# Linear-attention recurrence feeding a mixture of experts: state products on quarters of TensorE's array, and the low halves of w3 on GpSimd

## What is computed

```python
f = 1.0 / (1.0 + np.exp(-f_logit))          # q, k, v, f_logit: (4, 8, 768, 48)
for t in range(S):
    state = f[:, :, t, :, None] * state + np.einsum('bhd,bhe->bhde', k[:, :, t], v[:, :, t])
    y[:, :, t] = np.einsum('bhd,bhde->bhe', q[:, :, t], state)
```

## Time and profile before

| | us |
|---|---|
| median of three runs (728.39 to 729.1) | 728.86 |
| profiled execution | 729.75 |
| its span in the trace | 728.0 |
| end of the recurrence in the trace | 148.9 |
| TensorE busy | 714.8 |
| VectorE busy | 350.7 |
| ScalarE busy | 290.2 |
| GpSimd busy | 200.3 |

### The profile page before, as it was taken

How to read it: one execution, slowest core, us unless ns; L and a number is a source line. 1 busy time by engine, 2 the same in 40 slices (tenths; PEclk the granted TensorE clock), 3 DMA queues, 4 the chain that set the end, 5 groups by cost and what they waited for, 6 DMA issues and landing times.

```text
span 728.0 us, 14063 instructions
## 1 busy us (share of the span) xinstructions
PE 714.8 (98%) x4911; PEld 655.6 (90%) x4911; DVE 350.7 (48%) x580; ACT 290.2 (40%) x557; POOL 200.3 (28%) x234
## 2 busy tenths in 40 slices
PE   7999999999989999999999999999999999999997
PEld 6999899989989999999999988988988989889887
DVE  6889998768745545455465541211312113112121
ACT  5677788534235534345354442212123022031130
POOL 5756677502320120200000003114033042141242
PEclk9999999999999999999999999999999999999999
DMA  7687886234463454423342440000000000010001
GB/s 220 194 240 212 252 255 158 78 118 122 133 206 96 136 166 131 130 86 109 113 124 86 130 130 1 1 11 33 1 22 22 0 32 11 0 43 0 20 23 43
DMA packets 73057, 70.80 MB, mean 97 GB/s; under 512 B 20520, under 2 KB 61480, under 8 KB 73024
## 3 DMA queue, kind: packets, MB, share of 16 engines
q1 hardware_dynamic: 69952, 60.95, 28.3%
q0 software_dynamic: 3072, 9.44, 4.2%
HBM read 60.88 MB, written 9.49 MB: 97 GB/s over the span
## 4 chain that ended last, share of the span: by engine, by line
PE 82%; DMA 5%; issue 5%; POOL 4%; DVE 2%; SPq 1%; ACT 0%; POOLq 0%; ACTq 0%; DVEq 0%
PE bank L743 14%; PE bank L744 14%; PE bank L745 14%; PE b_a L743 9%; PE b_a L744 9%; PE b_a L745 9%; DMA e_all<-last_rows 4%; PE b_a L673 2%; PE bank L682 2%; PE bank L722 1%; PE bank L702 1%; PE bank L713 1%; POOL apart L554 1%; POOL xs L606 1%; PE bank L834 1%
## 5 line engine op out<-in xcount | busy, mean ns | idle before, releaser
L632 POOL TENSOR_TENSOR p_lo<-prod,p_hi 128x512 fp32r<-128x512 f32 x42 | 53.9, 1283 | 333.3 <-ACT p_hi L1116 333.3
L1113 ACT COPY a_sb<-b_a 128x512 f32<-128x512 f32 x48 | 28.2, 587 | 218.2 <-PE bank L745 218.2
L1494 DVE TENSOR_TENSOR prod<-bank,a_sb 128x512 f32<-128x512 f32 x48 | 33.2, 691 | 165.7 <-ACT a_sb L1113 165.7
L1450 DVE SCALAR_TENSOR_TENSOR h_lo<-b_a,h_hi 128x432 fp32r<-128x432 f32 x64 | 38.8, 607 | 97.2 <-ACT h_hi L1066 97.2
L1066 ACT ACTIVATE h_hi<-b_a 128x432 fp32r<-128x432 f32 x64 | 34.0, 532 | 124.3 <-PE b_a L745 124.0
L1141 DVE TENSOR_TENSOR w_lo<-w_raw,w_hi 128x768 fp32r<-128x768 f32 x72 | 67.9, 956 | 5.3 <-ACT w_hi L1032 1.2
L743 PE MATMUL bank<-h_hi,w_hi 128*128 128x432 f32 x192 | 69.9, 364 | 0.2
L745 PE MATMUL b_a<-x_hi,w_lo 128*128 128x432 f32 x192 | 68.7, 358 | 0.0
L744 PE MATMUL b_a<-x_lo,w_hi 128*128 128x432 f32 x192 | 68.7, 358 | 0.0
L744 PE MATMUL bank<-h_lo,w_hi 128*128 128x432 f32 x192 | 68.7, 358 | 0.0
L745 PE MATMUL bank<-h_hi,w_lo 128*128 128x432 f32 x192 | 68.7, 358 | 0.0
(11 more groups left out here) (226 smaller groups left out, 1540.3 us busy)
## 6 DMA issues: line engine op xcount, KB each, us to landing
w_raw<-sets SPq DMA_DIRECT2D x80, 192.0 KB, 3.5
w_raw<-sets SPq DMA_DIRECT2D x40, 384.0 KB, 4.2
ring_all<-qkvf SPq DMA_DIRECT2D x24, 384.0 KB, 4.1
ring_fc<-qkvf SPq DMA_DIRECT2D x24, 192.0 KB, 3.9
ring_all<-qkvf SPq DMA_DIRECT2D x24, 192.0 KB, 3.2
x_recurrence<-x_all SPq DMA_DIRECT2D x24, 192.0 KB, 3.5
w_sb<-w_t SPq DMA_DIRECT2D x8, 512.0 KB, 4.9
wo_sb<-w_out SPq DMA_DIRECT2D x8, 192.0 KB, 4.2
```

Of the source, the lines that this page charges most:

```text
L632: pool.tensor_tensor(p_lo[:, f, :], prod[:, f % 2, :], p_hi[:, f, :].bitcast(F32), ALU.subtract).then_inc(pl_done, 1)
L1113: act.copy(a_sb[:, f % 2, :], b_a[f % 2][:]).then_inc(as_done, 1)
L1450: dve.scalar_tensor_tensor(out=h_lo[:, f % 2, 0:SW], in0=b_h[f % 2][:, 0:SW], scalar=0.0, in1=h_hi[:, f % 2, 0:SW].bitcast(F32), op0=ALU.m ...
L1494: dve.tensor_tensor(prod[:, f % 2, :], b_b[f % 2][:], a_sb[:, f % 2, :], ALU.mult).then_inc(pr_done, 1)
```

## The change

The state products take a quarter of the array each, 64 rows and a column half, straight from `state`; `apart`, `half` and `e_half` are gone. y stands in two banks, b_y0 for pairs 0 and 1 and b_y1 for pairs 2 and 3, where in the second the heads of a pair change places (`y_place`), so that four neighbouring products (j = 0, 2, then 1, 3) use four different quarters. `pick` follows that. The update products lie in the rest of b_y1 (b_up) and come after the chunk products; carry stands at the head of VectorE's next step, and copy_yT waits for it. For the last tiles update (21 to 23), carry and decay (20 to 23) are left out. GpSimd makes w3_lo at the end of its step, VectorE keeps wo_lo, and ScalarE makes w3_hi where wo_hi was and wo_hi at the end. state_ready puts TensorE's waits ahead of the transposes.

```diff
-    apart = early("apart", [P, B, NP, 2, D])
-    half = early("half", [P, 2])
-    e_half = early("e_half", [P, NP, 2])
+    scratch = early("scratch", [P, 8 * NT * E])
...
+    b_y01 = ctx.enter_context(nc.psum_tensor("b_y01", [P, 2, 512], F32))
+    b_y0, b_y1 = b_y01[:, 0, :], b_y01[:, 1, :]
+    YB = NP // 2 * P
+    b_up = b_y1[:, YB:YB + NP * D]
+    bank = [ctx.enter_context(nc.psum_tensor(f"bank{n}", [P, 512], F32)) for n in range(4)]
+    b_cum, b_qT, b_kT, b_x = bank
+    b_y, b_s = b_y0, b_y1
+
+
+    def y_place(j, g):
+
+        if j < NP // 2:
+            return b_y0[g * HP:g * HP + D, j * P:(j + 1) * P]
+        return b_y1[(1 - g) * HP:(1 - g) * HP + D, (j - NP // 2) * P:(j - NP // 2 + 1) * P]
...
-            sp.dma_start(pick[h % 2 * HP:h % 2 * HP + D, h // 2, 2 * D:],
+            place = (h % 2 if h // 2 < NP // 2 else 1 - h % 2) * HP
+            sp.dma_start(pick[place:place + D, h // 2, 2 * D:],
...
-            pool.tensor_tensor(e_half[:], last.unsqueeze(2).to_broadcast([P, NP, 2]),
-                               half[:].unsqueeze(1).to_broadcast([P, NP, 2]), ALU.mult).then_inc(half_done, 1)
-            pool.tensor_tensor(state[:, r % 4], s_sum[:], last.unsqueeze(2).to_broadcast([P, NP, D]), ALU.mult)
-            pool.wait_ge(half_done, i + 1)
-            pool.tensor_tensor(apart[:, r % 4], s_sum[:].unsqueeze(2).to_broadcast([P, NP, 2, D]),
-                               e_half[:].unsqueeze(3).to_broadcast([P, NP, 2, D]), ALU.mult).then_inc(s_done, 1)
+            pool.tensor_tensor(state[:, r % 4], s_sum[:], last.unsqueeze(2).to_broadcast([P, NP, D]), ALU.mult
+                               ).then_inc(s_done, 1)
+
+        def low_w3(m, u):
+
+            rows = bass.ds(m * 2 - 2 + u // 2, 1)
+            cols, places = slice(u % 2 * FF // 2, (u % 2 + 1) * FF // 2), slice(u % 2 * KF // 2, (u % 2 + 1) * KF // 2)
+            by_place = lambda ap: ap.rearrange("p a (f n) -> p f (a n)", n=P)
+            pool.wait_ge(w3_hi_done, m * 8 + (2 * u - 7))
+            pool.tensor_tensor(w3_lo[:, places, rows, :].rearrange("p f a n -> p f (a n)"),
+                               by_place(w3_sb[:, rows, cols]), by_place(w3_hi[:, rows, cols].bitcast(F32)),
+                               ALU.subtract).then_inc(w3_lo_done, 1)
...
-            if (i := tile_of(s, -2)) is not None:
+            if (i := tile_of(s, -2)) is not None and not (isinstance(i, int) and i >= NT - B):
                 decay(i, r + 2)
             if (i := tile_of(s, 3, 3)) is not None:
                 clamp(i, r + 3)
             if (i := tile_of(s, 1)) is not None:
                 scale_q(i, r + 1)
+            if part:
+                low_w3(*part)
...
-        pool.memset(state[:], 0.0)
-        alone(pool.memset(half[:], 1.0))
-        alone(pool.affine_select(out=half[:, 0:1], in_=half[:, 0:1], compare_op=ALU.is_ge, fill=0.0, base=HP - 1,
-                                 pattern=[[0, 1]], channel_multiplier=-1))
-        alone(pool.affine_select(out=half[:, 1:2], in_=half[:, 1:2], compare_op=ALU.is_ge, fill=0.0, base=-HP,
-                                 pattern=[[0, 1]], channel_multiplier=1))
-        pool.memset(apart[:], 0.0).then_inc(pads_done, 1)
+        pool.memset(state[:], 0.0).then_inc(pads_done, 1)
+        pool.sem_inc(w3_lo_done, 2)
...
+        def state_ready(i):
+            need(pe, yT_done, i)
+            need(pe, sum_done, min(i, NT - B) if isinstance(i, int) else i)
+            need(pe, s_done, i - B + 1)
+
         def state_products(i, r):
-            need(pe, yT_done, i)
-            need(pe, s_done, i - B + 1)
-            for j in range(NP):
+            for j in (0, NP // 2, 1, NP // 2 + 1):
                 for g in range(2):
-                    mm = pe.matmul(b_y[g * HP:g * HP + D, j * P:(j + 1) * P], apart[:, r % 4, j, g, :],
-                                   qT[:, r % 2, j, :], start=(j == 0), stop=False, skip_group_check=True)
+                    mm = pe.matmul(y_place(j, g), state[g * HP:(g + 1) * HP, r % 4, j, :],
+                                   qT[g * HP:(g + 1) * HP, r % 2, j, :], start=(j % (NP // 2) == 0), stop=False,
+                                   skip_group_check=True)
             mm.then_inc(sp_done, 1)
 
         def update_products(i, r):
 
-            pe.wait_ge(v_landed[r % 4], (i - r % 4) * 4 + 16)
-            need(pe, sum_done, i)
+            pe.wait_ge(ks_done, i + 1)
             for j in range(NP):
                 for g in range(2):
                     h = 2 * j + g
-                    mm = pe.matmul(b_s[g * HP:(g + 1) * HP, j * D:(j + 1) * D], ks[:, r % 2, h, :],
+                    mm = pe.matmul(b_up[g * HP:(g + 1) * HP, j * D:(j + 1) * D], ks[:, r % 2, h, :],
                                    ring_v[:, r % 4, h * D:(h + 1) * D], start=True, stop=True)
             mm.then_inc(kv_done, 1)
 
         def chunk_products(i, r):
             pe.wait_ge(am_done, i + 1)
+            pe.wait_ge(v_landed[r % 4], (i - r % 4) * 4 + 16)
             for j in range(NP):
                 for g in range(2):
                     h = 2 * j + g
-                    mm = pe.matmul(b_y[g * HP:g * HP + D, j * P:(j + 1) * P], ring_v[:, r % 4, h * D:(h + 1) * D],
+                    mm = pe.matmul(y_place(j, g), ring_v[:, r % 4, h * D:(h + 1) * D],
                                    am[:, g, j, :], start=False, stop=True, skip_group_check=True)
...
-                pe.wait_ge(w3_lo_done, 4 * KF + 4)
+                pe.wait_ge(w3_lo_done, 2 * KF + 2)
+                pe.wait_ge(wo_lo_done, 2 * KF + 2)
...
+            if (i := tile_of(s, 0)) is not None:
+                state_ready(i)
...
                 state_products(i, r)
-                update_products(i, r)
                 chunk_products(i, r)
+                if not (isinstance(i, int) and i > NT - B):
+                    update_products(i, r)
...
         def copy_yT(i):
             act.wait_ge(y_done, i + 1)
+            if not isinstance(i, int) or i < NT - B:
+                act.wait_ge(sum_done, i + 1)
+            elif i == NT - B:
+                act.wait_ge(kv_done, i + 1)
             need(act, xl_at, i)
-            act.copy(yT[:], b_y[:]).then_inc(yT_done, 1)
+            act.copy(yT[:].rearrange("p (h n) -> p h n", h=2), b_y01[:, :, 0:YB]).then_inc(yT_done, 1)
...
         def high_wo(m, u):
             rows, half = bass.ds(m * 2 - 2 + u // 2, 1), slice(u % 2 * DM // 2, (u % 2 + 1) * DM // 2)
             act.wait_ge(w3_in[u // 2], m * 32)
-            act.wait_ge(w3_lo_done, m * 8 + (2 * u - 6))
+            act.wait_ge(wo_lo_done, m * 4 + (u - 3))
             act.copy(wo_hi[:, rows, half], wo_sb[:, rows, half]).then_inc(w3_hi_done, 1)
 
         def high_w3(m, u):
             rows, half = bass.ds(m * 2 - 2 + u // 2, 1), slice(u % 2 * FF // 2, (u % 2 + 1) * FF // 2)
+            act.wait_ge(w3_in[u // 2], m * 32)
+            act.wait_ge(w3_lo_done, m * 4 + (u - 3))
             act.copy(w3_hi[:, rows, half], w3_sb[:, rows, half]).then_inc(w3_hi_done, 1)
...
             if part:
-                high_wo(*part)
+                high_w3(*part)
...
             if part:
-                high_w3(*part)
+                high_wo(*part)
...
-            need(dve, kv_done, i - 1)
+            need(dve, kv_done, min(i - 1, NT - B + 1) if isinstance(i, int) else i - 1)
+            if isinstance(i, int) and i - 2 > NT - B:
+                dve.wait_ge(tr_done, i - 1)
...
-            dve.tensor_tensor(s_sum[:], state[:, r % 4], b_s[:, 0:NP * D].rearrange("p (j e) -> p j e", j=NP), ALU.add
+            dve.tensor_tensor(s_sum[:], state[:, r % 4], b_up.rearrange("p (j e) -> p j e", j=NP), ALU.add
...
-        def low_w3(m, u):
+        def low_wo(m, u):
 
             rows, half = bass.ds(m * 2 - 2 + u // 2, 1), slice(u % 2 * DM // 2, (u % 2 + 1) * DM // 2)
-            dve.wait_ge(w3_hi_done, m * 8 + (2 * u - 7))
-            low(wo_lo[:, rows, half], wo_sb[:, rows, half], wo_hi[:, rows, half]).then_inc(w3_lo_done, 1)
-            cols, places = slice(u % 2 * FF // 2, (u % 2 + 1) * FF // 2), slice(u % 2 * KF // 2, (u % 2 + 1) * KF // 2)
             dve.wait_ge(w3_hi_done, m * 8 + (2 * u - 6))
-            by_place = lambda ap: ap.rearrange("p a (f n) -> p f (a n)", n=P)
-            low(w3_lo[:, places, rows, :].rearrange("p f a n -> p f (a n)"), by_place(w3_sb[:, rows, cols]),
-                by_place(w3_hi[:, rows, cols])).then_inc(w3_lo_done, 1)
+            low(wo_lo[:, rows, half], wo_sb[:, rows, half], wo_hi[:, rows, half]).then_inc(wo_lo_done, 1)
 
         def step(s, r, part=None):
+            if (i := tile_of(s, -1)) is not None and not (isinstance(i, int) and i >= NT - B):
+                carry(i, r + 3)
...
-            if (i := tile_of(s, 0)) is not None:
-                carry(i, r)
             if (i := tile_of(s, 2)) is not None:
                 scale_k(i, r + 2)
             if part:
-                low_w3(*part)
+                low_wo(*part)
...
```

(23 more changed lines are left out.)

## The result

| | before | after |
|---|---|---|
| median of 20 runs each, us | 728.70 (726.70 to 729.43) | 731.11 (729.11 to 732.66) |
| profiled execution, us | 729.75 | 730.94 |
| its span | 728.0 | 729.1 |
| end of the recurrence | 148.88 | 151.78 |

The ratio is 1.0035, with an interval of 1.0026 to 1.0044: the change made the kernel slower by 0.35%, where 722.7 us was forecast and 728.4 was the upper end.

The account below looks back on a forecast made before the run. TensorE, 98% busy, was taken to bound the recurrence. Savings of 2.6 us (steps 5 to 20), 1.4 (0 to 4) and 2.2 (21 to 23), together 6.2, gave 722.7 us, range 719.5 to 728.4.

Parts of the forecast that it names:

- ks is done by 5.21: VectorE's step: ks finished 5.21 us into the step, from the 0.74 that sum and ks took together and kT's turn.
- The margin is 0.53, so the new wait is hidden while VectorE is on time: Copy of y, waiting for the sum, ends at 1.02 us; rows and logits want it at 1.55.
- D: Rival on TensorE: quarters sharing a bank don't overlap, state products take 1.09, step 5.90, 731.3 us; chance 0.09.
- E: Rival on the decays' round through DRAM: every round slow, step 6.1, 730.8 us; chance 0.08.
- B: Rival, clean: VectorE and GpSimd miss each other, step 5.44, 9.0 us saved, 719.9 us; chance 0.20.
- State products: TensorE: sixteen records four abreast take 0.635 us instead of 0.91, saving 0.28 a step.
- TensorE's floor: TensorE's own work in one step of the recurrence, falling from 5.72 to 5.44 us.
- The last three steps: Steps 21 to 23: shorter state products and dropped update products save 3 x (0.28 + 0.45) = 2.2 us.
- Steps 0 to 4: First five steps of the recurrence: 0.28 saved in each, 1.4 us together.
- The ring through wo_hi: Copy of y, weight halves, squares, wo_hi, wo_lo, sum: 5.33 us, about 5.44 with hand-overs; 0.15 for memory makes 5.59.
- 1.28 for its part: GpSimd: low_w3 takes 1.28 us, as p_lo of that size; qs is then ready by 7.33, wanted at 7.86.
- C, the lock: Rival: low_w3 holds VectorE back for its whole 1.28, step 5.88, 1.6 us faster, 727.3 us; chance 0.18.

Follow-up runs that it names:

- experiment 1: Kernel after, with ks made behind the sum on VectorE, at the head of the next step: 722.80 us, 0.9921 of the kernel before.
- experiment 2: Kernel after, with four buffers for ks instead of two and nothing moved: 724.33 us, 0.9947 of the kernel before.
- experiment 3: Kernel after, with the low half of w3 back on VectorE, between ks and wo_lo: 740.17 us (one run).
- experiment 10: Kernel before, with only the update products moved behind the chunk products: 728.21 us, 0.9996 of the kernel before.
- experiment 7: Kernel after, with ks behind the sum, wo_hi ahead of the squares and the low half of w3 back on VectorE: 719.23 us, 0.9879 of the kernel before.
- experiment 4: Kernel after, with SyncE's load of f for tile 4 ahead of the embedding's eight small loads: 731.33 us, 1.0039 of the kernel before.
- experiment 5: Kernel after, with ks behind the sum and, on ScalarE, wo_hi ahead of the squares: 721.75 us, 0.9906 of the kernel before.
- experiment 9: Kernel after, with ks behind the sum, wo_hi early, low half of w3 on VectorE and the early load of f: 720.37 us, 0.9890 of the kernel before.

## Why the prediction was wrong

**The step that failed** is in the part on VectorE: "ks is done by 5.21". I had timed ks by what stands ahead of it on VectorE and not by what it waits for. It needs a buffer that the update products of tile s free, and these end at 5.44 after the move. With it the sentence "The margin is 0.53, so the new wait is hidden while VectorE is on time" fell: the sum does not follow TensorE's end after 0.05 but after ks 0.59 and wo_lo 0.27 (start to start, 108.02 to 108.88), so the copy of y starts at 109.30 and not at about 108.2. From it on the step is fixed: 0.64 to the rows (109.30 to 109.94), and the rest of TensorE's step. 16 steps gave +5.5 in place of -2.6, and steps 0 to 4 lost their gain as well. Experiments 1 and 2, 8.3 and 6.8 us under the kernel after, show it by taking the coupling away in two ways, 3 by lengthening it, 10 by the move without it. Of the 0.68 that ks took, 0.12 is the clamp's by the estimate in experiment 3.

**Not among the rivals.** The result, 731.11, lay near D (731.3) and E (730.8), by chance, since neither was the cause: the state products took 0.59 (D decides above 0.91), and the whole list of waits from 82 to 140 us has none of the sum for GpSimd. B's step and time (5.44, 719.9) are nearly what experiment 7 shows, once ks is behind the sum and w3_lo back.

**State products** 0.635: measured 0.58 to 0.59. **TensorE's floor** 5.44: measured 5.44 in experiment 7. The Trainium skill (TensorEngine Tiling (Array Packing), Gotcha 1: PSUM Pressure) says that different row tiles cannot access the same PSUM bank simultaneously. These overlapped all the same, on different partitions of one bank: by that sentence no more than two of the four quarters could run at a time, and at the 0.114 a pair of the earlier trace rows that would take 0.91. Here the measurement decides.

**The last three steps** -2.2: measured -2.2 (13.37 against 15.59).

**Steps 0 to 4** -1.4: measured +1.6. With the early load (experiment 4) they took 27.95, so in that execution the load is the whole 1.6, and the gain of 1.4 had gone in the wait of ks: without that (experiment 1) they took 26.80 against 27.92, -1.1.

**The ring through wo_hi** with 0.15 for memory, 5.59: hidden behind ks in the kernel after, 5.66 in experiment 1. This term was right in kind and low by 0.07; wo_lo alone had 0.25 for memory there (0.59 against 0.34).

**GpSimd** 1.28 for its part: measured 1.40 on the median, by its row in all 16 steps:

```profile
L569 POOL TENSOR_TENSOR w_lo<-w_sb,w_hi x16: 1273/1405/1416, 44.8 to 136.5; - x16
```

The queue on GpSimd fitted, but the part did not pay: with the wait of ks gone, moving it back to VectorE gained 2.5 us (experiments 5 and 7; their intervals just overlap, and their steps are 5.55 and 5.44).

**C, the lock**, was not met in the form that the prediction gave it: lg_lo took 0.55 in all 16 steps, but it started 0.28 us or more ahead of GpSimd's part in each, so it never came second. Where a VectorE operation with two inputs in SBUF came second behind a GpSimd operation with two, it did wait for nearly the whole of it: ks in experiment 2 ended 0.41 after GpSimd's part (100.94 and 100.53) and wo_lo in experiment 5 ended 0.21 after the decay (105.24 and 105.03). Alone they take 0.55 and 0.34, so each had begun only some 0.14 before the other's end. Behind the clamp, which has one input, they waited less and ended before it did: ks 0.68 in the kernel after (108.70, the clamp 108.94), wo_lo 0.59 in experiment 1.

**The start** is no part of the change, see below.

**The stage behind the recurrence** changed its length by 1.8 us between the two profiles, over the 1 us that the prediction named as a sign of being wrong. It is not the change either: profiles of the changed kernels have both lengths, see below.

## What to carry to other kernels

When a step of one engine moves to the end, list for every buffer that it reads whose next writer now waits, and what stands behind that writer in its engine's list; the wait for a free buffer is as real as the one for data, and in a trace of before it shows nowhere. A double buffer that was refilled half a step early can be mended by a place further back in the list or by two more buffers. And relief of an engine that is full, but not late, was worth nothing here, while the engine that got the work handed it back with contention.

## What the runs showed of the hardware

**The start of TensorE.** The first running sum takes either 0.69 or 0.45 us for the same product. In the kernel before and after:

```profile
6.76 0.69 PE L664 MATMUL bank<-lg_hi,upto_r 128*128 128x384 f32 x1 [1.16 <-DVE lg_lo L1146]
```

```profile
6.33 0.45 PE L677 MATMUL bank<-lg_hi,upto_r 128*128 128x384 f32 x1 [0.73 <-DVE lg_lo L1173]
```

All profiles with 0.69 have the first scores at 12.7 to 13.6 us, and those with 0.45 or less at 11.3 to 11.5, but for experiment 9 at 12.18. Experiments 1 and 2 have the same text at the start and differ in this (13.47 and 11.52), so it is not the change. The granted clock reads 1.00 in both from 4 to 12 us, so the cause stays open. The two profiles of the kernel before and that of experiment 10 all had the slow one; whether it can have the other was not seen.

**Half clock behind the recurrence.** Some 12 us after its end, some executions have a stretch at the lower of the clock's two levels (1.2 in place of 2.4 GHz). The windows of TensorE there, before and then after (busy time, granted clock, DMA share, GB/s):

```profile
158.00:160.00 2.00, 0.70 (x5) 1.00 0.98 253
160.00:162.00 2.00, 1.89 (x9) 0.71 0.86 257
162.00:164.00 2.00, 2.00 (x7) 0.50 0.95 290
```

```profile
160.00:162.00 2.00, 1.55 (x9) 1.00 0.97 233
162.00:164.00 2.00, 1.01 (x7) 1.00 0.94 314
```

In the kernel before TensorE stood still for 1.4 us, busy for 0.70 of 2 us, ahead of the fall; in the kernel after it stood still for the same 1.4 us between 160 and 164, and the clock stayed. In the slow stretch products follow each other every 0.32 us instead of every 0.17. It costs some 1.4 us: behind the recurrence the nine profiles with it have 578.1 to 579.1 us (before 579.1) and the four without it 576.7 to 577.3 (after 577.3). Together with the start it makes profiles of one kernel differ by more than the 2.4 us between the medians, so steps of a stage had to be compared, not spans.
